# Two feed-forward layers on TensorE: the loop order of products and output banks in the down blocks

## The reference

```python
attn_out = _attn_ref(q, k, v, n_global, n_local)      # 4 batches, 8 heads, 768 positions, 64 wide
x = attn_out.transpose(0, 2, 1, 3).reshape(3072, 512)
# first layer:  w_in (512, 2048), w_out (2048, 512)
h = x @ w_in
x = (h * np.cos(h)) @ w_out
# second layer: other weights of the same sizes
h = np.maximum(x @ w_in, 0.0)
return (h * h @ w_out).astype(np.float32)
```

## Time and profile before

| | us |
|---|---|
| median of 3 runs | 1324.86 (1323.99 to 1330.97) |
| span of the profiled execution | 1324.0 |
| TensorE busy in it, 6256 matmuls | 1260.6 |
| VectorE busy | 641.6 |
| ScalarE busy | 506.0 |
| GpSimd busy | 218.0 |

### The profile page before, as it was taken

The page is one execution under the profiler, slowest core; times in us unless marked ns, Lnnn a source line. Parts: engine busy times, 40 slices in busy tenths (PEclk is TensorE's granted clock), DMA queues, the critical chain, the costliest instruction groups (busy, mean ns, idle before and its releaser), DMA issues.

```text
span 1324.0 us, 18435 instructions
## 1 busy us (share of the span) xinstructions
PE 1260.6 (95%) x6256; PEld 1001.7 (76%) x6256; DVE 641.6 (48%) x1454; ACT 506.0 (38%) x1110; POOL 218.0 (16%) x335
## 2 busy tenths in 40 slices
PE   4887887899999999999999999999999999999999
PEld 2666665688787787887887778888888888888887
DVE  5887886455656556556557762222222222222222
ACT  2666665444545444445445442221122222222211
POOL 1777776000000000000004880000000000000000
PEclk9999998899999999999999999999999999999999
DMA  4888897200300303003005333020020020200000
GB/s 110 206 212 217 208 223 206 90 0 1 127 1 13 116 0 114 16 0 127 0 1 183 103 113 110 0 96 1 1 96 0 21 75 0 95 0 0 32 1 32
DMA packets 132978, 97.61 MB, mean 74 GB/s; under 512 B 60064, under 2 KB 107296, under 8 KB 132896
## 3 DMA queue, kind: packets, MB, share of 16 engines
q1 hardware_dynamic: 132896, 96.56, 24.8%
HBM read 65.08 MB, written 31.46 MB: 73 GB/s over the span
## 4 chain that ended last, share of the span: by engine, by line
PE 82%; DVE 6%; issue 3%; ACT 2%; POOL 2%; SPq 2%; DMA 2%; DVEq 0%; ACTq 0%; POOLq 0%
PE psum L581 13%; PE psum L582 13%; PE psum L583 13%; PE psum L748 7%; PE psum L749 7%; PE psum L750 7%; PE psum L742 6%; PE psum L743 6%; PE psum L744 6%; POOL probs L527 2%; DMA w_stage<-in_moe_w_out_dram 1%; PE psum L630 1%; PE psum L650 1%; ACT probs L782 1%; DVE probs L943 1%
## 5 line engine op out<-in xcount | busy, mean ns | idle before, releaser
L1049 DVE TENSOR_TENSOR g_lo<-act_h,g_hi 128x512 fp32r<-128x512 f32 x192 | 139.7, 727 | 371.4 <-ACT g_hi L822 371.4
L581 PE MATMUL psum<-x_parts,w_in_hi 128*128 128x512 f32 x768 | 304.6, 397 | 4.6 <-issue 3.4
L582 PE MATMUL psum<-x_parts,w_in_hi 128*128 128x512 f32 x768 | 304.6, 397 | 0.0
L583 PE MATMUL psum<-x_parts,w_in_lo 128*128 128x512 f32 x768 | 304.5, 396 | 0.0
L837 ACT ACTIVATE act_h<-psum 128x512 f32<-128x512 f32 x96 | 57.3, 597 | 418.1 <-PE psum L583 418.1
L581 PEld LDWEIGHTS psum<-x_parts,w_in_hi 128*128 128x128 f32 x768 | 144.6, 188 | 39.6 <-issue 4.5
L582 PEld LDWEIGHTS psum<-x_parts,w_in_hi 128*128 128x128 f32 x768 | 144.6, 188 | 37.0 <-issue 1.5
L583 PEld LDWEIGHTS psum<-x_parts,w_in_lo 128*128 128x128 f32 x768 | 144.6, 188 | 35.2
L742 PE MATMUL psum<-g_hi,w_out_hi 128*128 128x512 f32 x384 | 153.0, 398 | 1.2 <-DVE g_lo L1049 1.2
L748 PE MATMUL psum<-w_out_hi,g_hi 128*128 128x512 f32 x384 | 152.2, 396 | 0.2 <-DVE g_lo L1049 0.2
L743 PE MATMUL psum<-g_lo,w_out_hi 128*128 128x512 f32 x384 | 152.0, 396 | 0.0
(11 more groups left out here) (79 smaller groups left out, 1510.6 us busy)
## 6 DMA issues: line engine op xcount, KB each, us to landing
w_stage<-in_moe_w_in_dram SPq DMA_DIRECT2D x32, 256.0 KB, 3.2
w_stage<-in_moe_w_out_dram SPq DMA_DIRECT2D x32, 256.0 KB, 2.9
raw<-in_q_dram SPq DMA_DIRECT2D x32, 192.0 KB, 3.3
raw<-in_k_dram SPq DMA_DIRECT2D x32, 192.0 KB, 3.8
x_hi_dram<-x_stage SPq DMA_DIRECT2D x48, 128.0 KB, 2.6
x_lo_dram<-x_stage SPq DMA_DIRECT2D x48, 128.0 KB, 3.0
x_parts<-x_hi_dram SPq DMA_DIRECT2D x6, 1024.0 KB, 6.3
x_parts<-x_lo_dram SPq DMA_DIRECT2D x6, 1024.0 KB, 8.4
```

The source lines that it names most:

```text
L581: pe.matmul(to, hi, x_parts[par][:, 0, c], start=(c == 0), stop=False)
L582: pe.matmul(to, hi, x_parts[par][:, 1, c], start=False, stop=False)
L583: last = pe.matmul(to, lo, x_parts[par][:, 0, c], start=False, stop=(c == KC - 1))
L1049: dve.tensor_tensor(g_lo[:, f % 2], act_h[:, f % 4], g_hi[:, f % 2].bitcast(F32), ALU.subtract).then_inc(g_lo_ready, 1)
```

## The change

In a down block the loop over the three products becomes the outer one, and that over the four banks the inner one. TensorE goes through the hi by hi product of banks 0 to 3, then the second product of all four, then the third. The accumulation starts and ends where it did for each bank, by flags that now also look at n. `down_done` is still counted at the third product of each bank, in the order of c. The waits for emptied banks at f = 0 now stand ahead of the first four products. No other block, no other engine's code and no buffer is touched.

```diff
-                for c in range(KC):
-                    if f == 0:
+                for n in range(3):
+                    for c in range(KC):
+                        if f == 0 and n == 0:
...
-                    to = psum[:, Y_BANK + c]
-                    one, end = f == 0, f == FC - 1
-                    if layer == 0:
-                        hi = w_out_hi[:, f, P * c:P * c + P]
-                        lo = w_out_lo[:, f, P * c:P * c + P]
-                        pe.matmul(to, hi, g_hi[:, f % 2], start=one, stop=False)
-                        pe.matmul(to, hi, g_lo[:, f % 2], start=False, stop=False)
-                        last = pe.matmul(to, lo, g_hi[:, f % 2], start=False, stop=end)
-                    else:
-                        hi = g_hi[:, f % 2, P * c:P * c + P]
-                        lo = g_lo[:, f % 2, P * c:P * c + P]
-                        pe.matmul(to, hi, w_out_hi[:, f], start=one, stop=False)
-                        pe.matmul(to, hi, w_out_lo[:, f], start=False, stop=False)
-                        last = pe.matmul(to, lo, w_out_hi[:, f], start=False, stop=end)
-                    last.then_inc(down_done, 1)
+                        to = psum[:, Y_BANK + c]
+                        cols = slice(P * c, P * c + P)
+                        one, end = f == 0 and n == 0, f == FC - 1 and n == 2
+                        if layer == 0:
+                            held = (w_out_hi, w_out_hi, w_out_lo)[n][:, f, cols]
+                            moved = (g_hi, g_lo, g_hi)[n][:, f % 2]
+                        else:
+                            held = (g_hi, g_hi, g_lo)[n][:, f % 2, cols]
+                            moved = (w_out_hi, w_out_lo, w_out_hi)[n][:, f]
+                        last = pe.matmul(to, held, moved, start=one, stop=end)
+                        if n == 2:
+                            last.then_inc(down_done, 1)
```

More of the change, by code:

```diff
@@ new lines, in down @@
+                for n in range(3):
+                    for c in range(KC):
+                        if f == 0 and n == 0:
+                            if layer == 0 and not is_tile(i, 0):
+                                pe.wait_ge(y_lo_ready, KC * (i - 1) + c + 1)
+                            if is_tile(i, TILES):
+                                pe.wait_ge(y_lo_ready, KC * (i - 1) + c + 1)
+                            elif layer == 1:
+                                pe.wait_ge(out_copied[c % 2], 2 * (i - 1 - TILES) + c // 2 + 1)
+                        to = psum[:, Y_BANK + c]
[10 more added lines that the diff above has]
+                            last.then_inc(down_done, 1)
```

## The result

The changed kernel took 1330.41 us (median of 20 runs) against 1326.19 us for the kernel before (20 runs, the three shown ahead of the prediction among them). The ratio is 1.0028 with a 95% interval of 1.0018 to 1.0039, which is 3.7 us more, 2.4 to 5.2 (the two medians lie 4.2 us apart). The forecast was 3.45 us more. The difference is less than the 0.5% which was set as the bound of no change, and clear of zero with this many runs.

The account below looks back on a forecast made before the run. The prediction took TensorE's 4608 product steps of 0.233 us as the bound; 0 + 1.4 + 0.65 + 1.4 + 0 = 3.45 us, added to the 1324.86 us median with 0.8 us of span difference, gave 1328.3 us, range 1324.2 to 1331.2.

Parts of the forecast that it names:

- (a) The steps: TensorE's steps inside down blocks: 1536 change kind by now crossing banks; claimed cost 0, with 1.7 us either way.
- (b) The boundaries of the first layer: Tiles 1 to 5: later banks delay g_lo and TensorE by 0.28 us each, 1.4 us in all (1.0 to 1.75).
- (b) The handover: First to second layer: g_lo starts 1.09 us later and ends 0.2 to 1.1 later; 0.65 us taken.
- the halving between two cases: Handover: 0.65 us as middle of 0.2 (GpSimd between pieces as g_lo runs) and 1.1 (same GpSimd load).
- (b) The boundaries of the second layer: Second-layer tile boundaries: g_lo ends near 879.85, TensorE wants it at 881.01; cost 0, or 0.15 each without cover.
- (b) The tail: Last tile's four stores: the train starts 1.40 us later, +1.4 us; ends 0.9 (closer stores pack better) and 1.5.
- (c) The waits at f = 0: First products of f = 0 down blocks, waits for four banks bunched within 4 steps: cost 0, at most 1.5 us.
- the engine likes the rotation: Rival on TensorE's steps: adding into the bank just written costs 0.018 us each, so 28 us would go, 1297 us; 2%.
- the copies' delay passes through everywhere: Rival at first-layer boundaries: each costs 1.09 us as at the handover, 7.9 us in all, 1332.8 us; 6%.
- The clock did not fall: Rival that the longer boundary hole drops TensorE's clock, all 192 down blocks costing 454 us more, 1779 us; 1%.
- nothing reaches the path: Rival: the tail's stores pack better and boundary delays are swallowed, +0.4 us or less, 1325 us; 13%.

Follow-up runs that it names:

- e1: The changed kernel with the down block of f = 15 back in the old bank-by-bank order; ratio to before 0.9992 (0.9982 to 1.0002).
- e3: The kernel before with VectorE's g_lo of f = 0 placed ahead of its copies out of the banks; ratio to before 0.9984 (0.9974 to 0.9995).
- e4: The changed kernel with VectorE's g_lo of f = 0 placed ahead of its copies out of the banks; ratio to before 1.0000 (0.9991 to 1.0009).
- e5: The kernel before with only the program's very last down block (tile 11, f = 15) in the new order; ratio to before 1.0009 (0.9999 to 1.0018).
- e2: The kernel before with the down block of f = 15 alone in the new order; ratio to before 1.0025 (1.0016 to 1.0034).
- e6: New order at f = 15 alone, without the last tile's store of bank 0; no ratio, span ends 4.63 us after the last product's start.
- e7: New order at f = 15 alone, without the last tile's store of bank 3; no ratio, span ends 4.34 us after the last product's start.

## Why the prediction was right, point by point

**(a) The steps.** Forecast 0, within 1.7 us. Right: 0.2331 to 0.2333 by the loads' rows after, and e1's 180 rotated blocks cost nothing that its interval or its trace shows. The reading that settled it beforehand was that the old order held both kinds of step and that the earlier trace rows tell them apart.

**(b) The boundaries of the first layer.** Forecast a step of 0.84 us in place of 0.56, measured 0.84. Over the five boundaries the trace gives 0.28, 0.28, 0.28, 0.28 and 0.22 more than before, in all 1.35 us, for the forecast's 1.4. What made the size come out was following the chain product, ScalarE, VectorE with the slack at each link. Of the 1.40 us by which bank 0 was late, VectorE's angle work swallowed all but 0.28. That it came out to the hundredth is luck: the last product of the block before starts at 335.84 + 0.70 = 336.54, so ScalarE began its copy 0.20 us before it, where the chain of the forecast had 0.27, and VectorE began 0.62 after ScalarE, where the forecast had 0.69. The two errors of 0.07 cancel. At the fifth boundary ScalarE does begin 0.27 before the product, and there the loss is 0.22. e3 and e4 show that the hole is g_lo standing behind four copies, since it goes when g_lo is moved.

**(b) The handover.** Forecast 0.65, measured 0.22 in the pair of profiles. The delay of g_lo's start was right, 1.1 us; what the halving between two cases could not give was how long g_lo would take. The trace after is at the low end that the prediction named, g_lo in 0.69 us. But the pair is one draw: e1 and e5, which empty the banks of f = 15 in the old order at this place too, have no hole there at all. In e5 g_lo is short as well:

```profile
786.92 0.68 DVE L1049 TENSOR_TENSOR g_lo<-act_h,g_hi 128x512 fp32r<-128x512 f32 x1
```

So the 0.55 of the kernel before went with its long g_lo and is no fixed cost of the old order. Where neither g_lo is stretched the step goes from 0.23 to 0.76 (e2) and the one after it by a further 0.1, together 0.6 us. And e6 and e7, which have the changed order at this place, have steps of 0.85 and 1.06. The rows of e7:

```profile
789.70 1.29 POOL L519 TENSOR_TENSOR w_in_lo<-w_stage,w_in_hi 128x512 fp32r<-128x512 f32 x1
...
790.56 0.98 DVE L1051 TENSOR_TENSOR g_lo<-act_h,g_hi 128x512 fp32r<-128x512 f32 x1
...
791.60 0.50 PE L751 MATMUL psum<-w_out_hi,g_hi 128*128 128x512 f32 x1 [0.66 <-DVE g_lo L1051]
```

So the term runs from 0.2 (the pair of profiles) to 0.9 (e7 against e1 or e5), and 0.65 lies inside by being a middle. What decides is the condition that the prediction named, whether GpSimd is at work as g_lo begins. GpSimd's subtraction ends at 790.99 in e7 and g_lo at 791.54, 0.55 us later; in the kernel before it is 790.73 and 791.27, in the changed one 791.31 and 791.85. It is the same in all nine traces. Of the g_lo that began while a GpSimd instruction was running, 97 in all, 92 ended 0.54 to 0.55 us after it, and the other five, for which that would have been sooner than their usual time, took 0.68 to 0.69. Where GpSimd began at the same time or later (38), g_lo took 0.68 to 0.69. That is a regularity of the rows; no run took GpSimd's work away.

**(b) The boundaries of the second layer.** Forecast 0. Right. VectorE in order of time and TensorE's next down block, after (they answer to the earlier trace rows):

```profile
878.62 1.29 DVE L1065 COPY y_stage<-psum 128x512 f32<-128x512 f32 x2 [5.45 <-PE psum L747]
879.83 0.68 DVE L1047 TENSOR_TENSOR g_lo<-act_h,g_hi 128x512 fp32r<-128x512 f32 x1
...
881.59 1.10 PE L747 MATMUL psum<-w_out_hi,g_hi 128*128 128x512 f32 x4
```

g_lo ends at 880.51, still 1.1 us ahead.

**(b) The tail.** Forecast 1.4, measured 1.29 (3.67 to 4.96). The start of the train came out: its first packet moves 1.40 us later. The difference lies in how the stores follow one another: before, they land 0.75, 0.71 and 0.66 us apart, after, 0.68, 0.67 and 0.66, so the train itself is some 0.1 us shorter. That before the second and third store waited a little for their copies fits this and is not shown. The prediction gave this as the reason of its low end.

**(c) The waits at f = 0.** Forecast 0, at most 1.5 us. Right: the fifth product of the block follows the first after 1.03 us, 0.33 and three steps.

**The sum.** The terms measured add up to 0 + 1.35 + 0.22 + 1.29 = 2.9 us, against 2.7 us of the pair of profiles from the second down block on. The rest is a hole in the middle of tile 5 that stands in one execution at 746 us and in the other at 763 us and is 0.2 us shorter there. The timed difference of 3.7 us (2.4 to 5.2) agrees with both. The predicted 1328.3 us was built on the 1324.86 us of three runs; over 20 runs the kernel before has 1326.19, and these 1.3 us, not a term, are most of the distance to 1330.41. The range of 1324.2 to 1331.2 held it, by 0.8 us.

**The rivals.** That the engine likes the rotation fell with (a). That the copies' delay passes through everywhere fell at the boundaries, where 0.28 of 1.09 came through. The clock did not fall: its mean over the span is 0.996 after and 0.993 before, and in none of the nine traces is the granted clock under 1.00 between 255 us and TensorE's last product, though the changed kernel's holes are 0.6 us long (0.84 less a step). That nothing reaches the path fell with the tail and the boundaries.

The version that beats both is e3, the old order with g_lo ahead of the copies: 0.9984 (0.9974 to 0.9995), about 2 us under the kernel before.

## What to carry to other kernels

When several accumulations share an engine, the order of the products is free in the middle and costs at the ends: what matters is when the first bank is finished, because the copies, and behind them the stores, start there. Count the steps by which each finished result moves and follow each reader with its slack; only the share that no other work swallows is paid. And look at what stands behind the copies on the copying engine, since moving that one instruction ahead gained about 2 us here (0.7 to 3.4 by its interval), where the boundaries had lost 1.35 by the change.

## What the runs showed of the hardware

- A 128x512 product of this type starts every 0.233 us at a granted clock of 1.00, whether it goes to the bank of the one before or to another, and whether its stationary tile is the same or a new one. The load of a tile held twice in a row is done twice, 188 ns each.
- A VectorE subtraction between SBUF tiles, 128x512, takes 0.68 us with GpSimd idle. While GpSimd splits the second layer's weights, between some 710 and 796 us, 8 to 13 of the 192 g_lo in an execution took 0.9 to 1.79 us. Those that began while a GpSimd instruction was running ended 0.54 to 0.55 us after it, and those that began first were not longer. At the handover g_lo took 1.56 us before, 0.69 in the changed kernel, 0.92 in e1, 0.68 in e2 and e5, 0.78 in e6 and 0.98 in e7. In the changed order this moved TensorE by 0.3 us (steps of 0.76 to 1.06), in the old one also by 0.3 (0.23 to 0.55), so a term of this size can't be forecast from one trace.
- Four stores of 256 KB behind one another keep the DMA engines 0.94 busy at about 350 GB/s. In both kernels the first packet moved 1.5 us after the first copy began, and the end of the span came 3.7 to 3.8 us after that.
